# One fused attention and mixture-of-experts kernel: last queries' scores in other PSUM banks, routing work and loads dealt anew

## What is computed

```python
scores = scale * q @ k.T                        # causal mask, softmax
local = softmax(scores) @ v
q_p = where(q > 0, q, exp(q) - 1) + 1
mem_out = (q_p @ M_prev) / (q_p . z_prev + 1e-6)
x = g * mem_out + (1 - g) * local               # g = sigmoid(beta), per head
logits = x @ w_gate;  e = argmax(logits)        # top 1 of 8
eom = sigmoid(x @ w_output_gate)
out = softmax(logits)[e] * eom[e] * (relu(x @ w1[e]) @ w2[e])
```

## Time and profile before

| | us |
|---|---|
| median of 3 runs | 502.44 (495.66 to 502.51) |
| the profiled execution | 499.52 |
| its span, first to last instruction | 497.8 |
| PE busy | 468.8 (94%) |
| DVE busy | 308.1 (62%) |
| ACT busy | 281.7 (57%) |
| POOL busy | 195.2 (39%) |

### The profile page before, as it was taken

One profiled execution on the slowest core, in us unless ns is written; L12 is line 12 of the kernel. 1 busy time (PEld: TensorE's weight loads), 2 busy tenths in 40 slices (PEclk: granted clock), 3 DMA queues, 4 the chain that ended last, 5 costly groups with the idle time before them and its releaser, 6 DMA issues.

```text
span 497.8 us, 11159 instructions
## 1 busy us (share of the span) xinstructions
PE 468.8 (94%) x3920; PEld 378.1 (76%) x3921; DVE 308.1 (62%) x783; ACT 281.7 (57%) x623; POOL 195.2 (39%) x187
## 2 busy tenths in 40 slices
PE   4999999998899797998999999999999999999995
PEld 3877778776667675886888888788888878878884
DVE  4388888998898896595222279922223983992221
ACT  5488888897888586336222248622224864862221
POOL 6547576676988766125222111121111112111100
PEclk9599999999999898999999999999999999999998
DMA  6324344496333715056222147951111694640000
GB/s 204 94 78 118 104 119 136 131 348 180 99 104 99 225 31 156 18 181 226 93 73 76 43 145 223 362 190 43 43 43 33 215 336 183 210 150 21 21 14 22
DMA packets 47359, 64.54 MB, mean 130 GB/s; under 512 B 9678, under 2 KB 28622, under 8 KB 47312
## 3 DMA queue, kind: packets, MB, share of 16 engines
q1 hardware_dynamic: 43232, 54.34, 33.9%
q0 software_dynamic: 4080, 9.60, 5.7%
HBM read 57.03 MB, written 10.90 MB: 136 GB/s over the span
## 4 chain that ended last, share of the span: by engine, by line
PE 76%; DVE 13%; issue 6%; DMA 3%; DVEq 1%; ACT 0%; POOL 0%; SPq 0%; ACTq 0%; POOLq 0%
PE S L1402 8%; PE O_ps L1574 8%; PE S L1574 8%; PE O_ps L1576 8%; PE S L1576 8%; PE O_ps L1575 8%; PE S L1575 7%; PE O_ps L1402 7%; DVE probs L940 4%; PE TP_ps L1601 4%; PE STK L1402 4%; PE TP_ps L1402 3%; PE STK L1565 2%; DMA v_nat<-in_v 2%; DVE w_lo L1152 1%
## 5 line engine op out<-in xcount | busy, mean ns | idle before, releaser
L1265 DVE TENSOR_TENSOR hid_lo<-TP_ps,hid_hi 128x512 fp32r<-128x512 f32 x46 | 31.8, 690 | 109.3 <-ACT hid_hi L851 97.1
L738 ACT ACTIVATE probs<-probs,neg_max 128x128 f32<-128x128 f32 (+2 forms) x144 | 82.9, 581 | 19.9 <-DVE neg_max L940 19.5
L686 POOL DMA_INDIRECT out<-x_ring,slot_tok_i x23 | 24.8, 1079 | 143.0 <-ACT x_ring L859 115.9
L1574 PE MATMUL S<-w_hi,x_hi 128*128 128x512 f32 x180 | 72.3, 402 | 0.0
L1576 PE MATMUL S<-w_hi,x_lo 128*128 128x512 f32 x180 | 70.4, 391 | 0.0
L1575 PE MATMUL S<-w_lo,x_hi 128*128 128x512 f32 x180 | 70.1, 390 | 0.0
L1574 PE MATMUL O_ps<-w_hi0b,hid_hi 128*128 128x512 f32 x152 | 62.9, 414 | 1.3 <-DVE hid_lo L1265 0.9
L608 POOL DMA_INDIRECT x_ring<-x_tokens,slot_tok_i x28 | 30.6, 1093 | 83.5 <-DMA out<-x_ring,slot_tok_i 72.0
L1576 PE MATMUL O_ps<-w_hi0b,hid_lo 128*128 128x512 f32 x152 | 59.5, 392 | 0.0
L1575 PE MATMUL O_ps<-w_lo0b,hid_hi 128*128 128x512 f32 x152 | 59.4, 391 | 0.0
L1152 DVE TENSOR_TENSOR w_lo<-w_raw,w_hi 128x1024 fp32r<-128x1024 f32 x44 | 51.3, 1217 | 10.5 <-ACT w_hi L767 10.5
(11 more groups left out here) (230 smaller groups left out, 945.7 us busy)
## 6 DMA issues: line engine op xcount, KB each, us to landing
w_raw<-in_moe_w SPq DMA_DIRECT2D x60, 512.0 KB, 4.8
q_pair<-in_qt SPq DMA_DIRECT2D x15, 288.0 KB, 2.9
k_pair<-in_kt SPq DMA_DIRECT2D x15, 288.0 KB, 3.1
v_nat<-in_v SPq DMA_DIRECT2D x16, 256.0 KB, 3.0
x_tokens<-x_out SPq DMA_DIRECT2D x16, 256.0 KB, 2.4
x_ring<-in_moe_w SPq DMA_DIRECT2D x3, 512.0 KB, 7.3
m_aug<-in_m_aug SPq DMA_DIRECT2D x1, 648.0 KB, 5.7
q_tail<-in_qt SPq DMA_DIRECT2D x32, 16.0 KB, 2.8
```

The costliest lines, as they stand in the source:

```text
L686: nc.gpsimd.indirect_dma_start(out=out[:, :], out_offset=bass.IndirectOffsetOnAxis(ap=slot_tok_i[:, t:t + 1], axis=0), in_=x_ring[:, t % X ...
L738: last = nc.scalar.activation(pr, pr, ACT.Exp, bias=neg_max[:, slot, h:h + 1], scale=-1.0, accum_out=sums[g % 2][:, at:at + 1])
L1265: V.tensor_tensor(hid_lo[:, 4 * f:4 * f + 4, :], TPB_ps[:, f, :].rearrange("r (c t) -> r c t", c=4), hid_hi[:, 4 * f:4 * f + 4, :].bitcast ...
L1574: T.matmul(dst, hi, part(i, k)[:, cols], start=first, stop=False)
```

## The change

The four PSUM banks S3 and O_ps become one stretch S4, and the last queries' scores lie in its last two banks, TAIL and the first 64 columns of O_ps. `scores(g+1, 0)` now waits for the copy of unit (g, 1) by DVE; `scores(g+1, 2)` waits for the masking of the last queries; `tail_scores(g)` waits for `copy_out(g-1)` between its two products, and `scores` no longer does. The router products of batches 0 to 2 are written to spare columns of O_ps inside `tail_scores`, in pairs 6, 7, 10 and 14. The router's weights (64 products, `router_weights`) come before the last queries' scores of pair 0, with their loads ahead of pair 1's. DVE's `dens` becomes a reduction over a sum and a constant 1e-9 beside it. `lanes` of all batches are on DVE; the routing pieces are dealt anew to the places ahead of and behind the last mask row; POOL's `bounded` waits for the next pair's first scores, and `low_ahead` is in pairs 9 to 12. Expert 0's weights are loaded two pieces a pair in pairs 8 to 11, behind V's load; expert 1's first four in pair 14, behind it too. At the end `early_table` stands after the last transposes, `early_tokens` after the copies; the last transposed unit goes to STK; `first_products` waits for `early_slots`.

```diff
-    sums = [A(f"sums{u}", [P, NSUM]) for u in range(2)]
+    sums = [A(f"sums{u}", [P, NSUM, 2]) for u in range(2)]
...
-    r_apart = A("r_apart", [P, TPB, P])
...
-    S3 = psum("S3", [P, 3 * 512])
+    S4 = psum("S4", [P, 4 * 512])
...
-    O_ps = psum("O_ps", [P, 512])
...
-    TAIL = S3[:, 1024:1536]
+    S3, TAIL, O_ps = S4[:, 0:1536], S4[:, 1024:1536], S4[:, 1536:2048]
+    LASTQ = S4[:, 1024:1024 + S]
...
-    placed = sem("placed")
-    lanes_apart = sem("lanes_apart")
...
-        both = STK[:, :, :] if k == 3 else low if k == 1 or unit == (G - 1, NU - 1) else TPB_ps[:, :, :]
+        both = STK[:, :, :] if k == 3 or unit == (G - 1, NU - 1) else low if k == 1 else TPB_ps[:, :, :]
...
-    RANKS, COUNTS = TAIL[:, P:P + TPB * E], TAIL[:, 2 * P:2 * P + E]
+    def ranks(b):
+        return (TAIL if b == LAST else O_ps)[:, P:P + TPB * E]
+    def counts(b):
+        return (TAIL if b == LAST else O_ps)[:, 2 * P:2 * P + E]
...
-    RANK_PAIR = {8: 0, 11: 1, LAST * NPAIR + 1: 2}
-    READS = {6: 1, 8: 2, 11: 3, LAST * NPAIR + 1: 4}
-    LOW_PAIR = {10: 0, 11: 1, 13: 2, 15: 3}
+    RANK_PAIR = {7: 0, 10: 1, 14: 2}
+    READS = {6: 1, 7: 2, 10: 3, 14: 4}
...
-            load_qk(1)
...
+            load_qk(1)
...
             for g in range(G + 2):
-                if g == NPAIR + 4:
-                    sp.wait_ge(order_done, 1)
-                    x = expert_at(0)
-                    for k in range(PC):
-                        load_piece(0, x, k)
                 for b in range(LAST):
...
-                if g >= G - 2:
-                    x = expert_at(1)
-                    for k in {G - 2: range(KD - 1), G - 1: (KD - 1,)}.get(g, ()):
-                        sp.wait_ge(lo_first, k + 1)
-                        load_piece(1, x, k)
                 if g > 0:
...
+                if g == G - 2:
+                    sp.wait_ge(lo_first, KD)
+                    x = expert_at(1)
+                    for k in range(KD):
+                        load_piece(1, x, k)
+                if 0 <= g - 8 < PC // 2:
+                    if g == 8:
+                        sp.wait_ge(order_done, 1)
+                    x = expert_at(0)
+                    for k in (2 * (g - 8), 2 * (g - 8) + 1):
+                        load_piece(0, x, k)
...
+                pool.wait_ge(scored, NS * g + len(SLOTS[0]))
...
-                pool.wait_ge(scored, NS * g + len(SLOTS[0]))
...
-            def lanes(b):
-                ts = slice(b * TPB, (b + 1) * TPB)
-                pool.wait_ge(r_consts_dve, 1)
-                pool.wait_ge(placed, b + 1)
-                nc.gpsimd.tensor_tensor(r_apart[:, :, :], iota_f[:, None, :].broadcast_to([P, TPB, P]),
-                                        r_lane[:, ts][:, :, None].broadcast_to([P, TPB, P]), ALU.subtract).then_inc(lanes_apart, 1)
-                pool.wait_ge(lanes_apart, b + 1)
-                nc.gpsimd.tensor_scalar(r_lanes[:, ts, :], r_apart[:, :, :], 0.0, None, ALU.is_equal).then_inc(lanes_done, TPB)
...
-                if g in LOW_PAIR:
-                    low_ahead(LOW_PAIR[g])
+                if 0 <= g - 9 < KD:
+                    low_ahead(g - 9)
                 if g == G - 1:
...
-                for b in range(LAST):
-                    if g == (9, 12, 14)[b]:
-                        lanes(b)
...
-                                                accum_out=sums[g % 2][:, at:at + 1])
+                                                accum_out=sums[g % 2][:, at, 0:1])
...
+                for u in range(2):
+                    V.memset(sums[u][:, :, 1], 1e-9)
...
-                V.tensor_copy(m_aug[:, :, D:HC], O_ps[:, 0:G * RE].rearrange("r (g e) -> r g e", e=RE)).then_inc(mw_copied, 1)
+                V.tensor_copy(m_aug[:, :, D:HC], O_ps[:, P:P + G * RE].rearrange("r (g e) -> r g e", e=RE)).then_inc(mw_copied, 1)
...
                 for h in range(n):
-                    rows = S3[:, 512:512 + S] if i == NT else score_rows(h if i == 0 else heads[0], i)
+                    rows = LASTQ if i == NT else score_rows(h if i == 0 else heads[0], i)
...
-                V.tensor_scalar(dens[:, :], sums[u][:, :], 1e-9, None, ALU.add).then_inc(summed, 1)
+                V.tensor_reduce(dens[:, :], sums[u][:, :, :], AX.X, ALU.add).then_inc(summed, 1)
...
+                dve.wait_ge(inverted, x + 1)
...
-            def choose(b):
-                ts = tiles_of(b)
...
+            def choose(b):
+                ts = tiles_of(b)
...
-                V.tensor_copy(s_cnt[:, :], COUNTS).then_inc(rank_read, 1)
+                V.tensor_copy(s_cnt[:, :], counts(0)).then_inc(rank_read, 1)
...
+            def turns():
...
-                sel = V.tensor_tensor(r_sel[:, ts, 0:E], RANKS.rearrange("r (t e) -> r t e", e=E), hot[:, ts, :], ALU.mult)
+                sel = V.tensor_tensor(r_sel[:, ts, 0:E], ranks(b).rearrange("r (t e) -> r t e", e=E), hot[:, ts, :], ALU.mult)
                 if b < 2:
...
-                    dve.wait_ge(rank_read, READS[(8, 11)[b]])
+                    dve.wait_ge(rank_read, READS[(7, 10)[b]])
...
-                    V.tensor_scalar(s_void[:, :], COUNTS, -1.0, float(EARLY_TILES * P), ALU.mult, ALU.add).then_inc(rank_read, 1)
+                    V.tensor_scalar(s_void[:, :], counts(b), -1.0, float(EARLY_TILES * P), ALU.mult, ALU.add).then_inc(rank_read, 1)
...
-                lane = V.scalar_tensor_tensor(r_lane[:, ts], r_tile_of[:, ts, E], -float(P), r_slot[:, ts], ALU.mult, ALU.add)
-                if b < LAST:
-                    lane.then_inc(placed, 1)
-                else:
-                    link(lane)
-            def last_lanes():
-                for t in range(LAST * TPB, TT):
+                link(V.scalar_tensor_tensor(r_lane[:, ts], r_tile_of[:, ts, E], -float(P), r_slot[:, ts], ALU.mult, ALU.add))
+            def lanes(b, first=0, end=TPB):
+                for t in range(b * TPB + first, b * TPB + end):
...
             def void_slots():
-                dve.wait_ge(rank_read, READS[LAST * NPAIR + 1])
+                dve.wait_ge(rank_read, READS[14])
...
-                link(V.tensor_scalar(t_part[:, :], COUNTS, P / 2 - 0.5, 1.0 / P, ALU.add, ALU.mult))
+                link(V.tensor_scalar(t_part[:, :], counts(LAST), P / 2 - 0.5, 1.0 / P, ALU.add, ALU.mult))
...
-                    choose(0)
                 elif g == 7:
-                    order()
+                    turns()
                 elif g == 8:
...
+                    place(0)
+                elif g == 9:
+                    scale(0)
+                elif g == 10:
+                    open_gate(1)
+                    so_far(1, 2)
+                elif g == 11:
+                    scale(1)
+                elif g == 13:
+                    largest(2)
+                elif g == 14:
+                    scale(2)
+                elif g == 15:
+                    early_tiles()
+                    lanes(2, 0, 3)
+            def routing_behind(g):
+                if g == 5:
+                    choose(0)
+                    so_far(0, 1).then_inc(first_hot, 1)
+                elif g == 6:
+                    read_counts()
+                    order()
+                elif g == 7:
+                    read_ranks(0)
+                    experts_in_order()
+                elif g == 8:
...
                 elif g == 9:
-                    scale(0)
-                    place(0)
+                    largest(1)
+                    choose(1)
                 elif g == 10:
-                    choose(1)
-                    open_gate(1)
+                    read_ranks(1)
+                    place(1)
                 elif g == 11:
-                    so_far(1, 2)
-                    scale(1)
+                    lanes(0)
                 elif g == 12:
-                    place(1)
+                    lanes(1)
                 elif g == 13:
-                    largest(2)
...
-                elif g == 14:
-                    scale(2)
-                    place(2)
-            def routing_behind(g):
-                if g == 5:
-                    so_far(0, 1).then_inc(first_hot, 1)
-                elif g == 6:
-                    read_counts()
-                elif g == 7:
-                    experts_in_order()
-                elif g == 8:
-                    read_ranks(0)
-                elif g == 9:
-                    largest(1)
-                elif g == 11:
-                    read_ranks(1)
-                elif g == 13:
...
                 elif g == 14:
-                    early_tiles()
+                    read_ranks(2)
+                    place(2)
+                elif g == 15:
+                    lanes(2, 3)
...
-                        early_tokens()
...
-                    if RANK_PAIR.get(g) == 2:
-                        read_ranks(2)
+                    if g == G - 1:
+                        early_tokens()
                 if g == 0:
...
-                        last_lanes()
+                        lanes(LAST)
...
```

(48 more changed lines are left out.)

## The result

| | before | after |
|---|---|---|
| median, us | 501.52 (495.66 to 502.51, 4 runs) | 481.46 (479.34 to 482.84, 4 runs) |
| the profiled execution | 499.52 | 479.34 |
| its span | 497.8 | 477.6 |

Medians and ranges here take in all executions, the ratios leave out those over 1.5% longer than the fastest of their kernel.

A forecast was written before the change was run, and what follows sets the result against it. Late pairs, with routing work and weight loads alongside, were taken to carry the open loss on PE, 10.58 us. 499.52 - 6.1 (pairs) + 0.8 (new wait) - 1.5 (start) - 2.5 (end) = 490.2 us; range 484 to 498.

The forecast's parts named there:

- rival D: Before the gathered tile: PE's clock falls in the 2 us stall, some 3 us come back; 493 us; chance 0.15.
- The start, -1.5: Pair 0: router weights' products put in front fill PE's 1.61 us wait; -1.5 us, bounds 0 and -2.5.
- the clock rises earlier: Pair 0: the -2.5 us bound of the start's term, in case PE's clock gets up sooner.
- Pairs 7 to 14, -6.1 and +0.8: Late pairs: 6.1 of 10.58 us excess goes; the new wait inside `tail_scores` costs 0.8 over 14 pairs.
- the leftover of 4.5: Late pairs: 4.5 of the 10.58 us over plain pairs stays; bounds 1 and 10.58.
- 2.1 for a full DVE: Six late pairs: routing exceeds DVE's room of 1.6 to 2 us by some 0.35 each, 2.1 in all.
- 2.4 for POOL's blocks: Pairs 9 to 12: two-input DVE operations wait for POOL, 0.5 to 1.5 us each in 9 and 10; 2.4 in all.
- The new wait for `copy_out`, +0.8: Inside `tail_scores`: PE waits for ACT's copy, 0.06 us in 14 pairs; +0.8, bounds 0 and +3.
- The end, -2.5: After pair 15: the 2.85 us V wait goes, PE stands 1.9 for the gather; -2.5, bounds -5 and +1.
- C, "all fits": Late pairs and end: blocks fall into DVE's waits, gather nearly in time, clock holds; 484.9 us; chance 0.17.
- B: Late pairs: DVE is their bound, 9 of the 10.58 us stay; 494.7 us; chance 0.22.
- E: Every pair: ACT becomes the pace through `copy_out` on PE's path; 503 us at 0.9 late; chance 0.04.

The follow-up runs named there:

- e1: Changed kernel with the router weights' products and their loads back behind pair 0's last transposes; 481.43 us.
- e2: Kernel before with the router weights' products ahead of pair 0's last queries' scores, loads ahead of pair 1's; 495.87 us, ratio 1.0007.
- e10: Changed kernel with routing work behind the last mask row moved ahead of it in pairs 5, 8, 9, 11, 12, 13; deadline stays lifted; 481.20 us.
- e11: Changed kernel with that routing work ahead of the mask row and first scores again waiting for the previous pair's last mask row; 488.42 us.
- e3: Changed kernel with the old load order: eight weight pieces ahead of V in pair 8, expert 1's ahead of V in pairs 14 and 15; 482.63 us.
- e16: Changed kernel with PE stalled behind each of pairs 3 to 14 until unit (g, 3) is copied; 505.01 us.
- e6: Changed kernel with `dens` as the old two-port addition instead of a reduction; 483.35 us.
- e4: Kernel before with a pair's V load ahead of the weight pieces in the queue; 495.75 us, ratio 0.9985.
- e8: Changed kernel with `early_tokens` between the copies of units (15, 2) and (15, 3) instead of behind both; 479.50 us.
- e17: The same kernel as e8, run again later; 481.04 us.
- e7: Changed kernel with POOL's `bounded` no longer waiting for the next pair's first scores (`phi` waits instead); 482.38 us.
- e12: Changed kernel with the old two-port `dens` and first scores again waiting for the previous pair's last mask row; 485.47 us.

## Why the prediction was wrong

**Two terms failed: the clock of the start, and what the late pairs would keep.** The profiled executions differ by 20.2 us where the sum has 9.3. Of the 10.9 between them the start has 4.5, the pairs 7 to 14 have 4.7, and the end 1.85, by the steps below.

*The clock.* The kernel before loses some 9.7 us to three falls in its profiled execution, half of the whole gain. By the five steps above it would take some 490 to 492 with an unbroken clock (an estimate), and the changed kernel takes 480. The sum had some of this without its name: 1.7 in pair 14's excess and 2.9 in the `values` of the end. For the start it had a bound of -2.5 and no term. I had the rows for it (and the first scores of 1.66 at 167.25), and used them only for the end and for rival D, as a danger to the changed kernel. I didn't ask what the clock already costs before.

By the steps of the sum:

- *The start, -1.5; it was -6.0.* The failed step is "the clock rises earlier", bounded at -2.5. In the profile of before, the products are at full rate by about 10 us (transposes of 0.26 to 0.31), stand for 1.61, and from 13.7 to 23.9 run at half: `w_pair` 3.60, the next first scores 1.65. I read the 3.60 as the price of the operation. It is 2.04 at full clock. How much of the 6.0 is the change's stays open, and much of it is scatter: pair 3 starts at 35.5 to 39.3 (median 36.6) in the sixteen profiles of the changed kernel and its variants, at 36.2 to 41.7 (median 38.9) in the four of the kernel before and its variants, of which the profile of before is the latest. Moving the weights, which I credited, shows nothing by itself in the medians (e1, e2).
- *Pairs 7 to 14, -6.1 and +0.8; it was -10.0.* The failed step is the leftover of 4.5: 2.1 for a full DVE and 2.4 for POOL's blocks came to 1.3 together. I gave DVE room for 1.6 to 2 us of routing. In pair 9 of the profile after it does 2.5 (from 108.21 to 109.54 ahead of the mask row, from 110.21 to 111.37 behind it), with the row done 0.12 behind the start of the next first scores, and the pair takes 10.56. That such a row may even start 0.6 behind them at no cost is the lifted deadline (e10). The two operations that POOL stretched in pairs 9 and 10 took 0.68 and 0.47, where I had blocks of 0.5 to 1.5. The new wait for `copy_out`, +0.8, is in the trace, as 0.57 on PEld in the row of a plain pair below, but nothing is lost on the products: a plain pair is 0.06 shorter, so this term was -0.7. Last, of before's 10.58, pair 14's 1.89 were not DVE's lateness but the clock: its first scores take 1.66 and its `local` 2.11 behind the wait of 2.80 that ended pair 13.

```profile
66.14 0.30 PEld L1402 LDWEIGHTS S<-k_pair,q_tail 128*128 128x128 f32 x2 [0.57 <-ACT out_T L746]
```

- *The end, -2.5; it was -4.35.* The stall for the gather came as foreseen, 1.06 instead of 1.9, since the gather landed 3.75 behind its issue where I took 4.9; that is 1.15 of the miss. The 0.5 taken for a fall of the clock was not needed: it held.
- *Right.* The wait for V in pair 9 is gone; `dens` is 0.16 throughout; no first scores wait for the mask row; the router weights start at 10.38 (forecast near 10.7); PE stands for the gather and otherwise for no more than 0.3 at the end. The token list was ready at T + 12.3, as computed. The deadline with the dealing, and the V load, are what the late pairs gained by; e11 and e3 bring back 5.7 and 1.8 of it.
- *The rivals.* C, "all fits", was nearest in mechanism and in time (484.9), and had 0.17. It was still 5.6 above the profiled execution, the start's clock for the most part. B fell with the late pairs, E with the plain ones. D looked for a fall of the clock in the changed kernel; the falls were in the kernel before. The base was not the cause: against the 497.18 of the later runs, 9.3 less is 487.9, and the changed kernel's ten runs have a median of 479.8.

The Trainium skill, "TensorE: Matmul & The Clock Gate", section "HAM oscillation — how this bites in real kernels", tells of PE stalls after which the array starts again at half clock, at a cost of half the throttled time. The case agrees on the price: nearly seven us at 0.50 cost 3.2 in e16. On when it happens, the counts above are what this case has.

The Trainium skill's rule on the shared port ("SBUF — State Buffer", "Who interferes with whom") is borne out by `dens` in e6, 1.64 beside `w_lo` and 0.16 as a reduction in the changed kernel. By that rule with one full block a pair I had 8 left in the late pairs; 1.3 were left, and no full block is in the trace: the longest, the 0.68 of pair 9, met only the last of `w_lo`.

## What to carry to other kernels

Before summing stalls, sum the clock: list the products that take more than their usual time, see which wait stands ahead of them, and price that loss as a term of its own. Removing one of two locks (a deadline, or the work ahead of it) can be worth nearly as much as removing both. A stall that is removed can come back at the next lock, as V's did in e4. Compare kernels by stretches of the trace that start behind the scattering part, not by totals that hold 3 us of scatter.

## What was not expected of the hardware

- The column of the granted clock reads 1.00 over the first 10 to 18 us even where the products plainly run at half rate (64 products in 3.60 instead of 2.04). The six slower of the twenty runs of the changed kernel, e8 and e17 show a mean clock of 0.998 or 0.999, the fourteen that are 3 us faster 0.995 to 0.998. At the start only the rows' own durations tell the clock.
- PE that was warmed with 24 products from 1.12 us on ran at full rate from about 7 us, and fell to half once more at 11.4, with no wait over 0.51 in between; in e10 it fell at 12.7, in e7 and e12 at 13.1 in the same way. Why is not settled.
- Five `lanes` of 128 columns beside a POOL operation of 1.65 us that had begun first took 1.66 instead of 1.07: a part of the time, not the whole of it.
